# Narrower first and last chunks of tokens in a two-layer MLP pipeline

## The chip, the cores and the metric

The kernel runs on one core of one Trainium2 chip. The metric is the device time of one execution in microseconds. Before the change it is 1582.55 us, the median of 3 runs (1582.0 to 1582.71).

## What is computed

Attention over pooled keys, and behind it two MLPs. There are 12288 query tokens of 128 channels and 768 pooled keys; all tensors are float32.

```python
kv_pool = kv.reshape(B, H // r, r, W // r, r, C).mean(axis=(2, 4))
k = v = kv_pool.reshape(B, -1, C) @ w_sr
s = scale * (q @ k.transpose(0, 2, 1))
a = softmax(s)                    # with 1e-9 in the denominator
x = a @ v                         # 12288 x 128
# MLP 1 (d_ff = 2048)
h = x @ w_in1;  x = (maximum(h, 0) ** 2) @ w_out1
# MLP 2 (d_ff = 2048): a rational function of h
h = x @ w_in2
P = a[0] + a[1]*h + a[2]*h**2 + a[3]*h**3
Q = 1.0 + abs(b[0])*abs(h) + abs(b[1])*h**2
out = (P / (Q + 1e-6)) @ w_out2
```

## The kernel before, in words

Channels lie on the 128 partitions and tokens along the free dimension, so x is a tile `X` of 128 x 12288 that stays in the on-chip memory from the attention to the end. The tokens are cut into `NCH` = 24 chunks of `T` = 512.

The attention stage (`step_a`, L154 and its callers) is done first, for all tokens. The change leaves it as it is. It ends about 297.6 us after the start of the span.

The MLP stage is one long loop, written out step by step, that every engine walks in its own order. A step is numbered `s`. The 2048 hidden features are `NF` = 16 blocks of 128, so a unit of work `t` is one block of one chunk: `t // NF` is its chunk, `t % NF` its block, and `NB` = 24 x 16 = 384 units make up each MLP. `LAG` = 21 is the number of steps by which MLP 2 runs behind MLP 1, since MLP 2 needs a whole chunk of MLP 1's output. The loop has `STEPS` = 384 + 21 + 6 steps. In step s:

- TensorE (PE) does, in this order: **H2**, three float32r matmuls for unit s-21 of MLP 2 (`three`, L534 to L538: high and low parts of weights and of x); **H1**, three for unit s of MLP 1; **ACC1**, one float32 matmul for unit s-2 that adds the squared block into the output of MLP 1 (L637); **ACC2**, the same for unit s-25 of MLP 2 (L646). A float32 matmul shows in the trace as two records.
- ScalarE (ACT): the square of unit s-2 where it is even (L372), `abs` (L377) and the product with a[3] (L378) of unit s-21, the logarithm (L384) of unit s-22, the `Relu` of unit s (L392), and the exponential (L398) of unit s-22. At chunk ends it also takes the accumulators out of PSUM: `x2h` (L359) and the output `osb` (L366). In steps 2 to 5 it rounds the four parts of `win2h` (L333).
- VectorE (DVE): five `scalar_tensor_tensor` instructions per unit: L502, L508, L513, L519, L526; of these L502, L513 and L526 belong to unit s-23, L508 to unit s-22 and L519 to unit s-21. At chunk ends it also makes `x1h` (L485) and `x2l` (L493).
- GpSimd (POOL): two instructions for unit s-21 (L278, L280) and the square of unit s where it is odd (L286). In steps 6 to 9 it makes the four parts of `win2l` (L245), and in the steps with s % 16 = 9 the next chunk's `x1l` (L261).

So steps 0 to 20 hold work of MLP 1 alone, steps 21 to 383 work of both, and from step 384 on work of MLP 2 alone. H1 has two PSUM buffers and H2 has four, so H2 of unit t waits until L526 of unit t-4 is done (`need(pe, g2_rdy, t - H2_RING + 1)`). Nothing is reordered at run time: every engine's list is fixed in the program, and semaphores hold an engine at its next instruction until its inputs are there. SyncE (SP) issues one output DMA for each chunk.

Of the kernel before, what the change touches and what calls it, by code (L numbers as in the profile page):

```python
# [30 lines left out]
def build_program(nc, qT, kvT, w_sr, w_in1, w_out1, w_in2, w_out2, coef_a, coef_b, outT):  # L31
# [25 lines left out]
    with ExitStack() as ctx:  # L57
# [234 lines left out]
        def _(act):  # L292
# [57 lines left out]
            for s in range(STEPS):  # L350
# [4 lines left out]
                if chunk_end(t):  # L355
# [3 lines left out]
                    nc.scalar.activation(x2h[:, c % 2, :], ACC1, ACT.Identity).then_inc(x2h_rdy, 1)  # L359

                t = s - LAG - 5
                if chunk_end(t):
# [3 lines left out]
                    nc.scalar.activation(osb[:, c % 2, :], ACC2, ACT.Copy, scale=-1.0).then_inc(o_rdy, 1)  # L366

                t = s - 2
                if in_b(t) and on_act(t):
# [2 lines left out]
                    nc.scalar.activation(g1[:, t % G_RING, :], r1[:, t % R_RING, :], ACT.Square).then_inc(sqa_rdy, 1)  # L372
# [300 lines left out]
```

## Time and profile before

| | |
|---|---|
| time, median of 3 | 1582.55 us |
| the profiled execution's own time | 1581.61 us |
| its span, first to last instruction | 1579.8 us |
| mean granted TensorE clock | 0.992 |
| busy over the span: PE, DVE, ACT, POOL | 95%, 94%, 86%, 72% |
| attention stage | 0 to 297.6 us |
| MLP stage, steps of MLP 1 alone | 297.6 to about 331.5 us |
| MLP stage, both | about 331.5 to about 1504 us |
| MLP stage, MLP 2 alone | to the end, 1579.8 us |

A busy share is the time in which an engine had at least one instruction recorded as running. Records of one engine overlap: a DVE instruction that is recorded with 0.74 us can be followed by the next one 0.66 us after its start. What an instruction costs in a full queue is therefore read as the distance from its start to the next start, here called its pitch, and not as its duration.

### The profile page before, as it was taken

What the parts mean: (1) busy time and instruction counts of PE and PEld (TensorE: products, weight loads), DVE (VectorE), ACT (ScalarE), POOL (GpSimd) and SP (SyncE); (2) the same over time, 40 slices, a digit from 0 to 9 for tenths busy, and PEclk for the clock granted to TensorE, in tenths of its full rate; (3) what the DMA queues carried; (4) which work ended last, traced back from release to release, by engine and by line L of the source; (5) the groups of instructions that cost most, each with busy time, mean ns of one, the idle gap of its engine ahead of it and who ended that gap; (6) DMA issues with size and microseconds to landing.
All of it is one profiled execution on the core that took longest, in us unless ns stands there. A gap on an engine that the chain in (4) does not pass through costs nothing.

```text
span 1579.8 us, 20254 instructions
## 1 busy us (share of the span) xinstructions
PE 1505.4 (95%) x5452; PEld 963.9 (61%) x5452; DVE 1483.9 (94%) x2591; ACT 1354.6 (86%) x2581; POOL 1141.0 (72%) x1119
## 2 busy tenths in 40 slices
PE   5999999999999999999999999999999999999975
PEld 4899999655555555555555555555555555555532
DVE  7888888359999999999999999999999999999998
ACT  3776777679999999999999999999999999999975
POOL 2544444467888878887888788878888788878864
PEclk9999999999999999999999999999999999999988
DMA  5100003000000000000000000000000000000000
GB/s 214 28 20 27 20 27 100 0 1 1 7 7 8 7 1 7 7 7 1 7 7 7 1 7 8 7 1 8 7 7 7 1 7 7 8 1 7 7 7 7
DMA packets 11223, 24.39 MB, mean 15 GB/s; under 512 B 1408, under 2 KB 1536, under 8 KB 10880
## 3 DMA queue, kind: packets, MB, share of 16 engines
q1 hardware_dynamic: 11136, 23.40, 4.4%
q8 instruction: 33, 0.54, 0.1%
q14 instruction: 54, 0.44, 0.1%
HBM read 17.11 MB, written 6.29 MB: 15 GB/s over the span
## 4 chain that ended last, share of the span: by engine, by line
DVE 69%; PE 19%; issue 10%; ACT 1%; POOL 1%; DMA 0%; SPq 0%; DVEq 0%; POOLq 0%; ACTq 0%
DVE tb L526 19%; DVE tb L508 16%; DVE tb L502 16%; DVE psum L513 15%; PE psum L596 6%; PE psum L571 6%; PE psum L582 4%; DVE tb L519 1%; DVE x2l L493 1%; PE psum L637 1%; DMA X<-kvT 0%; DVE x1h L485 0%; PE psum L555 0%; POOL pnorm L238 0%; PE psum L646 0%
## 5 line engine op out<-in xcount | busy, mean ns | idle before, releaser
L280 POOL TENSOR_TENSOR wb<-wb,ub 128x512 f32<-128x512 f32 x384 | 493.9, 1286 | 32.1
L278 POOL TENSOR_SCALAR wb<-ub,babs 128x512 f32<-128x512 f32 x384 | 297.7, 775 | 205.5 <-ACT ub L377 203.8
L637 PE MATMUL psum<-g,wout 128*128 128x512 f32 x768 | 403.8, 608 | 27.7 <-DVE x2l L493 25.1
L646 PE MATMUL psum<-tb,wout 128*128 128x512 f32 x768 | 398.2, 601 | 5.5 <-DVE tb L526 4.0
L519 DVE SCALAR_TENSOR_TENSOR tb<-tb,ca,psum 128x512 f32<-128x512 f32 x384 | 328.1, 854 | 7.0 <-ACT tb L378 7.0
L508 DVE SCALAR_TENSOR_TENSOR tb<-tb,ca,psum 128x512 f32<-128x512 f32 x384 | 328.0, 854 | 0.0
L502 DVE SCALAR_TENSOR_TENSOR tb<-tb,ca,psum 128x512 f32<-128x512 f32 x384 | 326.9, 851 | 0.1
L536 PE MATMUL psum<-x2h,win2h 128*128 128x512 f32 x384 | 302.4, 788 | 19.2 <-DVE tb L526 19.2
L513 DVE SCALAR_TENSOR_TENSOR psum<-wb,psum 128x512 f32<-128x512 f32 x384 | 307.8, 802 | 0.0
L526 DVE SCALAR_TENSOR_TENSOR tb<-psum,tb 128x512 f32<-128x512 f32 x384 | 305.9, 797 | 0.2
L377 ACT ACTIVATE ub<-psum 128x512 f32<-128x512 f32 x384 | 226.6, 590 | 54.5 <-PE psum L538 53.9
L398 ACT ACTIVATE psum<-lnb 128x512 f32<-128x512 f32 x384 | 232.3, 605 | 44.4 <-DVE tb L508 40.7
L378 ACT ACTIVATE tb<-psum,ca 128x512 f32<-128x512 f32 x384 | 261.4, 681 | 0.0
L646 PEld LDWEIGHTS psum<-tb,wout 128*128 128x128 f32 x768 | 147.3, 192 | 185.1 <-issue 170.1
L384 ACT ACTIVATE lnb<-wb 128x512 f32<-128x512 f32 x384 | 242.0, 630 | 0.0
L392 ACT ACTIVATE r<-psum 128x512 f32<-128x512 f32 x384 | 229.3, 597 | 13.1 <-PE psum L538 13.1
L286 POOL TENSOR_TENSOR g<-r 128x512 f32<-128x512 f32 x192 | 200.2, 1042 | 19.8 <-ACT r L392 19.8
L238 POOL TENSOR_SCALAR pnorm<-prob,stat 128x768 f32<-128x768 f32 x96 | 87.2, 908 | 143.9 <-DVE stat L454 143.8
L637 PEld LDWEIGHTS psum<-g,wout 128*128 128x128 f32 x768 | 134.6, 189 | 89.2 <-DVE x2l L493 35.1
L536 PE MATMUL psum<-x1h,win1h 128*128 128x512 f32 x384 | 158.4, 413 | 0.1
L538 PE MATMUL psum<-x2h,win2l 128*128 128x512 f32 x384 | 153.1, 399 | 0.0
L537 PE MATMUL psum<-x2l,win2h 128*128 128x512 f32 x384 | 152.9, 398 | 0.0
(64 smaller groups left out, 2147.3 us busy)
## 6 DMA issues: line engine op xcount, KB each, us to landing
qraw<-qT SPq DMA_DIRECT2D x25, 256.0 KB, 2.6
X<-kvT SPq DMA_DIRECT2D x16, 384.0 KB, 7.6
outT<-osb SPq DMA_DIRECT2D x24, 256.0 KB, 2.0
wraw<-w_in SPq DMA_DIRECT2D x2, 1024.0 KB, 10.9
wsr<-w_sr SPq DMA_DIRECT2D x1, 64.0 KB, 1.9
wout<-w_out SPq DMA_DIRECT2D x2, 0.5 KB, 8.2
ca<-coef_a SPq DMA_DIRECT2D x1, 2.0 KB, 2.1
cb<-coef_b SPq DMA_DIRECT2D x1, 1.0 KB, 2.2
```

What stands on the lines that cost most here:

```text
L278: nc.gpsimd.tensor_scalar(w, u, babs[:, 1:2], babs[:, 0:1], ALU.mult, ALU.add).then_inc(v_rdy, 1)
L280: nc.gpsimd.tensor_tensor(w, w, u, ALU.mult).then_inc(w_rdy, 1)
L378: nc.scalar.activation(tb[:, t % T_RING, :], H2[t % H2_RING], ACT.Identity, scale=ca[:, 3:4]).then_inc(t1_rdy, 1)
L384: nc.scalar.activation(lnb[:, t % LN_RING, :], wb[:, t % W_RING, :], ACT.Ln, bias=Q_ONE).then_inc(ln_rdy, 1)
L502: nc.vector.scalar_tensor_tensor(out=y, in0=y, scalar=ca[:, 0:1], in1=r, op0=ALU.add, op1=ALU.mult).then_inc(y_rdy, 1)
L508: nc.vector.scalar_tensor_tensor(out=p, in0=p, scalar=ca[:, 1:2], in1=H2[t % H2_RING], op0=ALU.add, op1=ALU.mult).then_inc(t3_rdy, 1)
L513: nc.vector.scalar_tensor_tensor(out=r, in0=wb[:, t % W_RING, :], scalar=Q_ONE, in1=r, op0=ALU.add, op1=ALU.mult).then_inc(e_rdy, 1)
L519: nc.vector.scalar_tensor_tensor(out=p, in0=p, scalar=ca[:, 2:3], in1=H2[t % H2_RING], op0=ALU.add, op1=ALU.mult).then_inc(t2_rdy, 1)
L526: nc.vector.scalar_tensor_tensor(out=y, in0=H2[t % H2_RING], scalar=-2.0, in1=y, op0=ALU.add, op1=ALU.mult).then_inc(g2_rdy, 1)
L536: mm(out, lh, rh, start=start, stop=False)
L637: mm(ACC1, wout1[:, f, :], g1[:, t % G_RING, :], start=(f == 0), stop=(f == NF - 1))\
L646: mm(ACC2, wout2[:, f, :], tb[:, t % T_RING, :], start=(f == 0), stop=(f == NF - 1))\
```

## The change

The MLP stage gets a list of chunk widths `CW` and of their offsets `CO`. The first and the last chunk are 256 tokens wide, the 23 between are 512 wide; there are `NC` = 25 chunks and `NB` = 400 units per MLP. All 12288 tokens are still covered, since 256 + 23 x 512 + 256 = 12288. `LAG` stays 21. Every instruction of a unit works on `n = CW[t // NF]` columns of its buffer, and the buffers keep their size. The attention stage still makes chunks of 512, so chunk c of the MLP stage, which now begins 256 tokens earlier, waits for the attention chunk that holds its last token.

```diff
-    NB = NCH * NF
+    CW = [T // 2] + [T] * (NCH - 1) + [T // 2]
+    CO = [sum(CW[:c]) for c in range(len(CW))]
+    NC = len(CW)
+    NB = NC * NF
...
-            for c in range(NCH):
+            for c in range(NC):
                 sp.wait_ge(o_rdy, c + 1)
-                sp.dma_start(outT[:, c * T:(c + 1) * T], osb[:, c % 2, :]).then_inc(o_out[c % 2], 16)
+                sp.dma_start(outT[:, CO[c]:CO[c] + CW[c]], osb[:, c % 2, 0:CW[c]]).then_inc(o_out[c % 2], 16)
...
-                nc.gpsimd.tensor_tensor(x1l[:, c % 2, :], X[:, c * T:(c + 1) * T], x1h[:, c % 2, :].bitcast(F32),
+                n = CW[c]
+                nc.gpsimd.tensor_tensor(x1l[:, c % 2, 0:n], X[:, CO[c]:CO[c] + n], x1h[:, c % 2, 0:n].bitcast(F32),
                                         ALU.subtract).then_inc(x1_rdy, 1)
...
                 if in_b(t) and not on_act(t):
-                    r = r1[:, t % R_RING, :]
+                    n = CW[t // NF]
+                    r = r1[:, t % R_RING, 0:n]
                     pool.wait_ge(r1_rdy, t + 1)
                     need(pool, g1_used, t - G_RING + 1)
-                    nc.gpsimd.tensor_tensor(g1[:, t % G_RING, :], r, r, ALU.mult).then_inc(sqp_rdy, 1)
+                    nc.gpsimd.tensor_tensor(g1[:, t % G_RING, 0:n], r, r, ALU.mult).then_inc(sqp_rdy, 1)
...
-                dve.wait_ge(x_rdy, c + 1)
+                dve.wait_ge(x_rdy, -(-(CO[c] + CW[c]) // T))
...
                 t = s - LAG - 2
                 if in_b(t):
-                    y = tb[:, t % T_RING, :]
+                    n = CW[t // NF]
+                    y = tb[:, t % T_RING, 0:n]
                     dve.wait_ge(y_rdy, t + 1)
                     dve.wait_ge(e_rdy, t + 1)
-                    nc.vector.scalar_tensor_tensor(out=y, in0=H2[t % H2_RING], scalar=-2.0, in1=y,
+                    nc.vector.scalar_tensor_tensor(out=y, in0=H2[t % H2_RING][:, 0:n], scalar=-2.0, in1=y,
                                                    op0=ALU.add, op1=ALU.mult).then_inc(g2_rdy, 1)
...
-                    three(H2[t % H2_RING], win2h[:, f:f + P], win2l[:, f:f + P],
-                          x2h[:, c % 2, :], x2l[:, c % 2, :]).then_inc(h2_rdy, 1)
+                    three(H2[t % H2_RING][:, 0:n], win2h[:, f:f + P], win2l[:, f:f + P],
+                          x2h[:, c % 2, 0:n], x2l[:, c % 2, 0:n]).then_inc(h2_rdy, 1)
```

All other instructions of the units on ACT, DVE, POOL and PE are narrowed in the same way.

On POOL, this is the list of steps 0 to 14, where MLP 1 runs alone. `g` is the square of an odd unit, `win2l` a part of MLP 2's weights, `x1l` the low part of the next chunk's x. Before:

```order
L261 TENSOR_TENSOR x1l<-X,x1h 128x512
L286 TENSOR_TENSOR g_83<-r_82 128x512 x3
L245 TENSOR_TENSOR win2l<-wraw,win2h 128x512
L286 TENSOR_TENSOR g_83<-r_82 128x512
L245 TENSOR_TENSOR win2l<-wraw,win2h 128x512 x2
L261 TENSOR_TENSOR x1l<-X,x1h 128x512
L286 TENSOR_TENSOR g_83<-r_82 128x512
L245 TENSOR_TENSOR win2l<-wraw,win2h 128x512
```

The same place on POOL after:

```order
L265 TENSOR_TENSOR x1l<-X,x1h 128x256
L292 TENSOR_TENSOR g_83<-r_82 128x256 x3
L248 TENSOR_TENSOR win2l<-wraw,win2h 128x512
L292 TENSOR_TENSOR g_83<-r_82 128x256
L248 TENSOR_TENSOR win2l<-wraw,win2h 128x512 x2
L265 TENSOR_TENSOR x1l<-X,x1h 128x512
L292 TENSOR_TENSOR g_83<-r_82 128x256
L248 TENSOR_TENSOR win2l<-wraw,win2h 128x512
```

The order is the same; the squares are 256 wide, the weight parts and the second chunk's `x1l` are as wide as before.

On PE, this is step 25, in which all four kinds of matmul appear for the first time. Before:

```order
L536 MATMUL psum<-x2h_84,win2h_52 128x512
L537 MATMUL psum<-x2l_85,win2h_52 128x512
L538 MATMUL psum<-x2h_84,win2l_53 128x512
L536 MATMUL psum<-x1h_60,win1h_50 128x512
L537 MATMUL psum<-x1l_61,win1h_50 128x512
L538 MATMUL psum<-x1h_60,win1l_51 128x512
L637 MATMUL psum<-g1_83,wout1_54 128x512
L646 MATMUL psum<-tb_81,wout2_55 128x512
```

The same step on PE after:

```order
L554 MATMUL psum<-x2h_84,win2h_52 128x256
L555 MATMUL psum<-x2l_85,win2h_52 128x256
L556 MATMUL psum<-x2h_84,win2l_53 128x256
L554 MATMUL psum<-x1h_60,win1h_50 128x512
L555 MATMUL psum<-x1l_61,win1h_50 128x512
L556 MATMUL psum<-x1h_60,win1l_51 128x512
L658 MATMUL psum<-g1_83,wout1_54 128x512
L668 MATMUL psum<-tb_81,wout2_55 128x256
```

In steps 21 to 36 the matmuls of MLP 2 belong to the narrow first chunk, while those of MLP 1 belong to 512-wide chunks (from step 16 on; ACC1, which is two steps behind, from step 18 on).

On DVE, the instructions of the last two units at the end of the program before, and then after:

```order
L508 SCALAR_TENSOR_TENSOR tb_81<-tb_81,ca_57,psum 128x512
L513 SCALAR_TENSOR_TENSOR psum<-wb_79,psum 128x512
L526 SCALAR_TENSOR_TENSOR tb_81<-psum,tb_81 128x512
L502 SCALAR_TENSOR_TENSOR tb_81<-tb_81,ca_57,psum 128x512
L513 SCALAR_TENSOR_TENSOR psum<-wb_79,psum 128x512
L526 SCALAR_TENSOR_TENSOR tb_81<-psum,tb_81 128x512
```

```order
L523 SCALAR_TENSOR_TENSOR tb_81<-tb_81,ca_57,psum 128x256
L529 SCALAR_TENSOR_TENSOR psum<-wb_79,psum 128x256
L544 SCALAR_TENSOR_TENSOR tb_81<-psum,tb_81 128x256
L516 SCALAR_TENSOR_TENSOR tb_81<-tb_81,ca_57,psum 128x256
L529 SCALAR_TENSOR_TENSOR psum<-wb_79,psum 128x256
L544 SCALAR_TENSOR_TENSOR tb_81<-psum,tb_81 128x256
```

The last 16 units are 256 wide, and 16 units of five instructions have come in over the whole list.

## Rows read from the trace of the kernel before

**Rows 1.** The chain that ended last, from the page: shares of the span by engine:

```profile
DVE 69%; PE 19%; issue 10%; ACT 1%; POOL 1%; DMA 0%; SPq 0%; DVEq 0%; POOLq 0%; ACTq 0%
```

**Rows 2.** Busy time by stretch (window, length, busy us and instructions per engine, clock, DMA):

```profile
297.60:334.00 36.40, 34.43 (x111) 20.18 (x109) 0.69 (x1) 21.91 (x40) 16.98 (x16) 1.00 0.00 0
...
334.00:1516.00 1182.00, 1152.10 (x3644) 678.23 (x3643) 1181.14 (x1874) 1101.81 (x2057) 964.50 (x939) 1.00 0.02 6
```

**Rows 3.** Timeline of DVE, one step (start, duration, engine, line, instruction, idle before):

```profile
340.95 0.74 DVE L502 SCALAR_TENSOR_TENSOR tb<-tb,ca,psum 128x512 f32<-128x512 f32 x1
...
342.26 0.69 DVE L513 SCALAR_TENSOR_TENSOR psum<-wb,psum 128x512 f32<-128x512 f32 x1
...
342.86 0.74 DVE L519 SCALAR_TENSOR_TENSOR tb<-tb,ca,psum 128x512 f32<-128x512 f32 x1
...
344.12 0.73 DVE L502 SCALAR_TENSOR_TENSOR tb<-tb,ca,psum 128x512 f32<-128x512 f32 x1
```

**Rows 4.** Timeline of PE, start of the MLP stage, MLP 1 alone:

```profile
297.57 0.40 PE L536 MATMUL psum<-x1h,win1h 128*128 128x512 f32 x1
...
306.14 1.02 PE L637 MATMUL psum<-g,wout 128*128 128x512 f32 x2
...
307.23 0.40 PE L537 MATMUL psum<-x1l,win1h 128*128 128x512 f32 x1
...
307.70 1.02 PE L637 MATMUL psum<-g,wout 128*128 128x512 f32 x2
...
331.50 0.80 PE L536 MATMUL psum<-x2h,win2h 128*128 128x512 f32 x1
```

**Rows 5.** Timeline of DVE, its first unit and its seventeenth:

```profile
334.01 0.75 DVE L519 SCALAR_TENSOR_TENSOR tb<-tb,ca,psum 128x512 f32<-128x512 f32 x1 [6.24 <-ACT tb L378]
...
384.66 0.75 DVE L519 SCALAR_TENSOR_TENSOR tb<-tb,ca,psum 128x512 f32<-128x512 f32 x1
```

**Rows 6.** Timeline of POOL, steps 7 to 11 (parts of win2l, x1l, squares):

```profile
311.12 2.51 POOL L245 TENSOR_TENSOR win2l<-wraw,win2h 128x512 fp32r<-128x512 f32 x2
...
314.83 1.03 POOL L286 TENSOR_TENSOR g<-r 128x512 f32<-128x512 f32 x1
```

**Rows 7.** Groups of instructions by line and shape: busy us, mean ns | idle before:

```profile
L280 POOL TENSOR_TENSOR wb<-wb,ub 128x512 f32<-128x512 f32 x384 | 493.9, 1286 | 32.1
...
L278 POOL TENSOR_SCALAR wb<-ub,babs 128x512 f32<-128x512 f32 x384 | 297.7, 775 | 205.5 <-ACT ub L377 203.8
...
L311 ACT ACTIVATE pth<-psum 128x384 fp32r<-128x384 f32 x192 | 84.0, 489 | 76.1 <-PE psum L582 76.0
...
L359 ACT ACTIVATE x2h<-psum 128x512 fp32r<-128x512 f32 x24 | 14.0, 582 | 0.3 <-PE psum L637 0.3
```

**Rows 8.** Timeline of PE in the attention stage, narrower matmuls (128x384, 128x128):

```profile
283.88 0.51 PE L571 MATMUL psum<-kh,ql 128*128 128x384 f32 x2
284.23 0.82 PE L582 MATMUL psum<-ident,pnorm 128*128 128x128 f32 x6
284.80 0.48 PE L596 MATMUL psum<-pth,vh 128*128 128x512 f32 x1
```

**Rows 9.** Timeline of DVE ahead of the attention stage, narrower instructions:

```profile
18.66 0.55 DVE L412 TENSOR_TENSOR kl<-psum,kh 128x384 fp32r<-128x384 f32 x1
...
19.12 0.55 DVE L415 TENSOR_TENSOR vl<-psum,vh 128x384 fp32r<-128x384 f32 x1
```

**Rows 10.** Busy time by stretch, near the end, MLP 2 alone:

```profile
1510.00:1512.00 2.00, 0.80 (x2) 0.00 (x0) 2.00 (x5) 1.13 (x3) 0.93 (x1) 1.00 0.00 0
...
1516.00:1518.00 2.00, 1.99 (x4) 1.49 (x5) 2.00 (x4) 1.04 (x3) 1.31 (x2) 0.50 0.00 0
```

**Rows 11.** Timeline of all engines, the last two rows that set the end:

```profile
1573.83 0.69 DVE L526 SCALAR_TENSOR_TENSOR tb<-psum,tb 128x512 f32<-128x512 f32 x1
...
1576.68 0.60 ACT L366 ACTIVATE osb<-psum 128x512 f32<-128x512 f32 x1 [4.99 <-PE psum L646]
```

More of the change, by code:

```diff
@@ L270, in _ @@
             for s in range(STEPS):
-                if s % NF == 9 and s // NF + 1 < NCH:
+                if s % NF == 9 and s // NF + 1 < NC:
                     split_x1(s // NF + 1)
@@ L358, in _ @@
                     need(act, h2_rdy, (c - 1) * NF)
-                    nc.scalar.activation(x2h[:, c % 2, :], ACC1, ACT.Identity).then_inc(x2h_rdy, 1)
+                    nc.scalar.activation(x2h[:, c % 2, 0:CW[c]], ACC1[:, 0:CW[c]], ACT.Identity).then_inc(x2h_rdy, 1)
                 t = s - LAG - 5
@@ L365, in _ @@
                     need(act, o_out[c % 2], c // 2 * 16)
-                    nc.scalar.activation(osb[:, c % 2, :], ACC2, ACT.Copy, scale=-1.0).then_inc(o_rdy, 1)
+                    nc.scalar.activation(osb[:, c % 2, 0:CW[c]], ACC2[:, 0:CW[c]], ACT.Copy, scale=-1.0).then_inc(o_rdy, 1)
                 t = s - 2
@@ L371, in _ @@
                     need(act, g1_used, t - G_RING + 1)
[L372 removed]
+                    n = CW[t // NF]
+                    nc.scalar.activation(g1[:, t % G_RING, 0:n], r1[:, t % R_RING, 0:n], ACT.Square).then_inc(sqa_rdy, 1)
                 t = s - LAG
@@ L383, in _ @@
                     act.wait_ge(w_rdy, t + 1)
-                    nc.scalar.activation(lnb[:, t % LN_RING, :], wb[:, t % W_RING, :], ACT.Ln,
+                    n = CW[t // NF]
+                    nc.scalar.activation(lnb[:, t % LN_RING, 0:n], wb[:, t % W_RING, 0:n], ACT.Ln,
                                          bias=Q_ONE).then_inc(ln_rdy, 1)
@@ L397, in _ @@
                     act.wait_ge(ln_rdy, t + 1)
-                    nc.scalar.activation(H2[t % H2_RING], lnb[:, t % LN_RING, :], ACT.Exp,
+                    n = CW[t // NF]
+                    nc.scalar.activation(H2[t % H2_RING][:, 0:n], lnb[:, t % LN_RING, 0:n], ACT.Exp,
                                          scale=-1.0).then_inc(r_rdy, 1)
@@ L492, in _ @@
                     dve.wait_ge(x2h_rdy, c + 1)
-                    nc.vector.tensor_tensor(x2l[:, c % 2, :], ACC1, x2h[:, c % 2, :].bitcast(F32),
+                    n = CW[c]
+                    nc.vector.tensor_tensor(x2l[:, c % 2, 0:n], ACC1[:, 0:n], x2h[:, c % 2, 0:n].bitcast(F32),
                                             ALU.subtract).then_inc(x2_rdy, 1)
-                if s % NF == 7 and s // NF + 1 < NCH:
+                if s % NF == 7 and s // NF + 1 < NC:
                     split_x1(s // NF + 1)
@@ L625, in _ @@
                     need(pe, r1_rdy, t - H1_RING + 1)
-                    three(H1[t % H1_RING], win1h[:, f:f + P], win1l[:, f:f + P],
-                          x1h[:, c % 2, :], x1l[:, c % 2, :]).then_inc(h1_rdy, 1)
+                    three(H1[t % H1_RING][:, 0:n], win1h[:, f:f + P], win1l[:, f:f + P],
+                          x1h[:, c % 2, 0:n], x1l[:, c % 2, 0:n]).then_inc(h1_rdy, 1)
                 t = s - 2
@@ L636, in _ @@
                     pe.wait_ge(sqa_rdy if on_act(t) else sqp_rdy, t // 2 + 1)
-                    mm(ACC1, wout1[:, f, :], g1[:, t % G_RING, :], start=(f == 0), stop=(f == NF - 1))\
+                    n = CW[t // NF]
+                    mm(ACC1[:, 0:n], wout1[:, f, :], g1[:, t % G_RING, 0:n], start=(f == 0), stop=(f == NF - 1))\
                         .then_inc(g1_used, 1)
@@ L645, in _ @@
                     pe.wait_ge(g2_rdy, t + 1)
-                    mm(ACC2, wout2[:, f, :], tb[:, t % T_RING, :], start=(f == 0), stop=(f == NF - 1))\
+                    n = CW[t // NF]
+                    mm(ACC2[:, 0:n], wout2[:, f, :], tb[:, t % T_RING, 0:n], start=(f == 0), stop=(f == NF - 1))\
                         .then_inc(g2_used, 1)
```

38 lines of the change are left out of this document (24 added, 14 removed).

## The prediction

> **What bounds the kernel now.** I read the page first: in the chain that ended last, DVE has 69% and PE 19% [rows 1]. A share over the whole span mixes stages, so next I read the busy time by stretch. The reader is to see two regimes there [rows 2]. From 297.6 to 334.0 DVE is busy for 0.69 us of 36.4 and PE for 34.4: while MLP 1 runs alone, PE sets the time. From 334 to 1516 DVE is busy for 1181.1 of 1182.0 us: from there on it never waits. The timeline of DVE gives the price of one step: from one L502 to the next 3.17 us, with five instructions in it [rows 3]. L502 and L508 together take 1.31, that is 0.655 each (L519 alike), and L513 takes 0.60 (L526 alike); 3 x 0.655 + 2 x 0.60 = 3.17. PE alone takes 307.70 - 306.14 = 1.56 us for a step with one H1 and one ACC1 [rows 4]. From L637 to L537 is 1.09, a float32 matmul and one float32r matmul; two float32r ones take 0.47. So a float32r matmul of 512 columns costs 0.235 and a float32 one 0.86. A step with all four kinds is 3.12 us of PE against 3.17 of DVE. The two are nearly even in the middle, and only DVE's price counts there. No wait is worth removing in the middle; what can move is the fill, the drain, and the number of instructions.
>
> I call 297.57, the first H1 [rows 4], zero. H2 of unit 0 starts at 33.9 [rows 4]. DVE starts at 36.4, 2.5 later, and handles unit 16, the first of the second chunk, at 384.66 - 297.57 = 87.1 [rows 5]. From there both versions have the same 368 units of 512 columns, 3.17 us each, DVE without a gap. So the sum has four terms: when DVE reaches unit 16, the 16 new units behind the 368, the new chunk end, and the tail behind DVE.
>
> **Prices at 256 columns,** which the trace doesn't show.
> - DVE: two instructions at 384 columns start 0.46 apart [rows 9], the like at 512 takes 0.60, so 128 columns cost 0.14, about DVE's 1.04 ns per column. The rest, 0.07 (0.12 where a column of coefficients is read), stays: 0.655 - 0.267 = 0.39 and 0.33, a step 3 x 0.39 + 2 x 0.33 = 1.83. Bounds: 1.585 if all of it halved, 2.0 if each keeps 0.04 more.
> - PE: at 384 columns two float32r matmuls take 284.23 - 283.88 = 0.35, so 0.175 each; six of 128 columns, each with its own weights, take 0.57, so 0.095 each [rows 8]. A line through 512 and 384 gives 0.12 at 256; ends 0.107 (streaming alone) and 0.175 (as dear as 384). Float32: half of 0.86 and a little, 0.44. An H1 plus ACC1 step: 3 x 0.12 + 0.44 = 0.80.
> - POOL: L278 and L280 take 0.78 + 1.29 = 2.06 at 512 [rows 7]; at 256 between 1.03 and 2.06. I take 1.5; it stays under DVE's 1.83. A square costs 1.03 [rows 6], at 256 between 0.52 and 1.03; I take 0.60, near the lower end, since no POOL row shows a fixed part of more than a few tenths.
> - ACT: 582 - 489 = 93 ns per 128 columns [rows 7], so 0.19 per instruction. In the middle it is busy for 1101.8 us in some 366 steps [rows 2], 3.0 a step.
>
> **The fill, steps 0 to 20.** PE's own work falls: H1 16 x 0.36 + 5 x 0.70 = 9.3, ACC1 16 x 0.44 + 3 x 0.86 = 9.6, together 18.9 against 31.0 before (21 x 0.70 + 19 x 0.86). But POOL's list doesn't shrink with it: four `win2l` parts and the second chunk's `x1l` stay 512 wide, 1.24 us each ((314.83 - 311.12) / 3) [rows 6], all in steps 6 to 9. Before, they lay beside 1.56 us steps. Now PE comes to step 5 at about 3.2 of work + 1.4 of the same starting waits = 4.6, and POOL starts the square of unit 5 some 0.8 later, at 5.4. Then: square 0.60, part 1.24, square 0.60, parts 2.48, `x1l` 1.24, square of unit 9 0.60: 12.2. Another part and the square of unit 11: 14.0. ACC1 of unit 9 stands in step 11, where PE is at 4.6 + 6 x 0.80 + 0.36 = 9.8: it waits about 2.4 us, and everything on PE behind it waits too. From ACC1 of unit 11: 14.0 + 0.44, two narrow steps 1.6, two steps of a wide H1 and a narrow ACC1 2.3, step 18 with the wait for the first `x2l` 2.0, two wide steps 3.1. H2 of unit 0 starts at 23.4 instead of 33.9.
>
> **A clock term.** In the tail of before, PE was busy for 0.80 of 2.0 us and the granted clock then was 0.50, that is 1.2 instead of 2.4 GHz, in a stretch 4 us later [rows 10]. The new wait leaves a like hole in front of PE-bound work. I add 1.5 us: some 3 us of PE work at half speed. Bounds 0 and 3.4.
>
> **Steps 21 to 36, narrow MLP 2 beside wide MLP 1.** Before, DVE set 3.17. Now DVE needs only 1.83, but PE still has a wide H1 and ACC1: 0.36 + 0.70 + 0.86 = 1.92, and 0.44 more in the 12 steps with ACC2. That is 30.7 + 5.3 = 36.0. I add 0.7 for the chunk end in step 34, where ACC1 waits for `x2l` and no DVE backlog hides it any longer, and 0.5 for the start. H2 of unit 16 starts at 23.4 + 37.2 = 60.6, with the clock term 62.1, and DVE has it at 64.6 instead of 87.1: **-22.5**. ACT lies below: 3.0 - 4 x 0.19 = 2.25 a step. What is late next is PE, and DVE idles for some 9 us here. That is the heart of it: the half-width units save time on an engine that has nothing else to do in these steps.
>
> **The 16 new units.** DVE has them behind the 368: 16 x 1.83 = **+29.3**. Beside it lie PE (0.80 a step; 1.6 even at 1.2 GHz) and POOL (1.5). Seen over both ends, DVE does 32 narrow units for 16 wide ones: 58.6 for 50.7 us, 7.9 us of fixed cost.
>
> **The new chunk end.** One narrow `x1h` and one narrow `x2l` more on DVE: **+0.6**. Output DMAs: one more, hidden.
>
> **Behind DVE.** From L526's end, 1574.52, to `osb` at 1576.68 PE does one float32 matmul at the low clock [rows 10, 11]. Half the columns save about 0.9 there and 0.2 in `osb`, and the last transfer may gain 0.1: **-1.2**.
>
> Sum: -22.5 + 29.3 + 0.6 - 1.2 = +6.2. The profiled execution took 1581.6, 0.9 less than the median of 1582.55, so it becomes 1587.8, and the median 1588.8. I forecast 1588.8 us, **slower**; with its bounds 1586 to 1592.
>
> **A rule weighed.** PE's weight loads overlap its streaming in these rows: 0.235 for 512 columns leaves no room for a load beside 0.213 of streaming, and 128 columns with their load take 0.095 [rows 4, 8]. The Trainium skill (TensorE: Matmul & The Clock Gate, Part 3, The mechanism) says that a LDWEIGHTS overlaps matmuls in flight only when it goes to another row group, and gives 128 columns of weights about 107 ns; by it every narrow matmul would pay its load, which I estimate from that figure at some 9 us more. The rows of 512 and 384 columns speak against it, since their matmuls would have to show the same load.
>
> **Rivals.**
> - *The fill gives all it can* (not slower). It decides at POOL's list in steps 6 to 9: if squares and weight parts come through in time there (a square well below 0.60, parts started earlier because `win2h` is there early), PE never waits at step 11. H2 of unit 0 comes at 18.9 + 1.4 + 0.4 = 20.7, the clock stays, and if steps 21 to 36 have no waits either, the sum is 6.2 - 2.7 - 1.5 - 1.2 = +0.8: 1583.4, no change. For it: PE's floor really falls by 12 us. Against it: 1.24 x 5 us stand in POOL's list whatever the width. To come out faster by over 3.2 us, DVE's step at 256 would have to be under 1.6 as well, which [rows 9] speak against.
> - *The narrow step is set by POOL or ACT*. If L278 and L280 hardly shrink (2.06), the last 16 units cost 16 x 0.23 = 3.7 more and steps 21 to 36 up to 2.06 + 0.52 = 2.6 instead of 2.25, 5 more: 1597.5. For it: no POOL row has another width in the same form. Against it: POOL's L245, L261 and L280 all take 1.24 to 1.29 at 512, as work by the column would.
> - *A narrow matmul pays its load*. If the 0.095 of 128 columns is all load and comes on top at 256, the five loads of a step's narrow part (three for H2, two for ACC2) cost 5 x 0.08 = 0.4; 16 x 0.4 in steps 21 to 36 and 1.5 in the fill behind the POOL wait: 8 more, 1596.8. The tail hides it (1.2 under 1.83).
>
> **How the numbers follow.** Forecast and its bounds 0.60; fill gives all 0.20; POOL or ACT 0.12; loads 0.05; anything else, either way, 0.03. A difference below 0.2% (3.2 us) can't be told from none. Faster (under 1579.4) needs the first rival and a cheaper DVE at once: 0.06. Within 0.2% (to 1585.7): most of the first rival and the low edge of the forecast, 0.19. Slower: 0.75. The range 1583 to 1596 leaves out under 1 in 10 at each side.
>
> **What would show it.** Right: H2's first matmul about 23 to 25 us after the first H1, a PE wait of 2 to 3 us for a POOL square in step 11; in steps 21 to 36 DVE with idle time of some 9 us and PE without; a DVE step of 1.8 us in the last 16 units without idle time; wide steps in the middle unchanged at 3.17. Wrong: a DVE step at 256 columns below 1.6 or above 2.0, no PE wait in the fill, a PE step above 2.4 in steps 21 to 36, or a middle that differs from 3.17 per unit.

## The result, and the profile after

The changed kernel took 1586.49 us (median of 9 runs, 1585.51 to 1587.35), the kernel before 1581.47 (median of 9 beside them, 1581.22 to 1582.71). The ratio is 1.0031, with a 95% interval of 1.0022 to 1.0040: slower by 5.0 us. The forecast was 1588.8 us, slower, with 1583 to 1596 as the range. The profiled execution took 1585.51 us with a span of 1583.7 us and a mean TensorE clock of 0.994.

The chain of the changed kernel gives DVE less and waiting for issue more than [rows 1]:

```profile
DVE 66%; PE 19%; issue 12%; ACT 1%; POOL 1%; DMA 1%; SPq 0%; DVEq 0%; POOLq 0%; ACTq 0%
```

Times below are counted from the first H1, as in the prediction. It starts at 296.76 in this execution, at 297.57 in the one before [rows 4]. First the fill, the steps in which MLP 1 runs alone. The timeline of PE after (start, duration, instruction, idle before in brackets) has the first H1, the wait in step 11, H2 of unit 0 and H2 of unit 16, the first of a 512-wide chunk:

```profile
296.76 0.28 PE L554 MATMUL psum<-x1h,win1h 128*128 128x256 f32 x1
...
307.68 0.28 PE L556 MATMUL psum<-x1h,win1l 128*128 128x256 f32 x1
309.72 0.70 PE L658 MATMUL psum<-g,wout 128*128 128x256 f32 x2 [1.77 <-POOL g L292]
...
320.89 0.68 PE L554 MATMUL psum<-x2h,win2h 128*128 128x256 f32 x1
...
357.36 0.58 PE L554 MATMUL psum<-x2h,win2h 128*128 128x512 f32 x1
```

H2 of unit 0 starts at 24.1 instead of 33.9, H2 of unit 16 at 60.6. PE stands still for 1.77 us at the square of unit 9. The timeline of POOL over the same steps, against [rows 6], shows why: the squares have shrunk, the parts of `win2l` and the second chunk's `x1l` have not.

```profile
302.96 0.61 POOL L292 TENSOR_TENSOR g<-r 128x256 f32<-128x256 f32 x1 [1.74 <-PE psum L658]
303.53 1.28 POOL L248 TENSOR_TENSOR win2l<-wraw,win2h 128x512 fp32r<-128x512 f32 x1
304.80 0.61 POOL L292 TENSOR_TENSOR g<-r 128x256 f32<-128x256 f32 x1
305.37 2.52 POOL L248 TENSOR_TENSOR win2l<-wraw,win2h 128x512 fp32r<-128x512 f32 x2
307.84 1.26 POOL L265 TENSOR_TENSOR x1l<-X,x1h 128x512 fp32r<-128x512 f32 x1
309.06 0.61 POOL L292 TENSOR_TENSOR g<-r 128x256 f32<-128x256 f32 x1
```

Next steps 21 to 36. The windows of the changed kernel (length, then busy time of PE, PE weight loads, DVE, ACT, POOL, clock, DMA) have a third regime between the two of [rows 2]: from 322 to 360 PE is full and DVE is not. From 360 on DVE never waits, as before.

```profile
322.00:360.00 38.00, 37.89 (x158) 26.21 (x157) 31.79 (x79) 34.34 (x91) 30.52 (x43) 1.00 0.00 1
360.00:1500.00 1140.00, 1112.74 (x3541) 656.93 (x3540) 1139.86 (x1810) 1062.98 (x1989) 930.38 (x906) 1.00 0.02 6
```

One step of this regime on PE and on DVE. PE's pitch, from H2 to H2, is 335.90 - 333.56 = 2.34. DVE has the same pitch (338.49 - 336.14), with a pause in each step:

```profile
333.56 0.47 PE L554 MATMUL psum<-x2h,win2h 128*128 128x256 f32 x1
333.86 0.28 PE L555 MATMUL psum<-x2l,win2h 128*128 128x256 f32 x1
333.98 0.28 PE L556 MATMUL psum<-x2h,win2l 128*128 128x256 f32 x1
...
335.65 0.59 PE L668 MATMUL psum<-tb,wout 128*128 128x256 f32 x2
335.90 0.47 PE L554 MATMUL psum<-x2h,win2h 128*128 128x256 f32 x1
```

```profile
336.14 0.48 DVE L516 SCALAR_TENSOR_TENSOR tb<-tb,ca,psum 128x256 f32<-128x256 f32 x1 [0.25 <-ACT psum L410]
...
337.42 0.48 DVE L536 SCALAR_TENSOR_TENSOR tb<-tb,ca,psum 128x256 f32<-128x256 f32 x1
...
338.49 0.48 DVE L516 SCALAR_TENSOR_TENSOR tb<-tb,ca,psum 128x256 f32<-128x256 f32 x1 [0.25 <-ACT psum L410]
...
359.65 0.75 DVE L536 SCALAR_TENSOR_TENSOR tb<-tb,ca,psum 128x512 f32<-128x512 f32 x1 [0.83 <-ACT tb L387]
```

The last row is unit 16 on DVE, at 359.65 - 296.76 = 62.9, against 87.1 before [rows 5]: 24.2 us earlier.

In the middle nothing moved: from the `x2l` of one chunk to that of the next it takes 51.66 us on average, and 51.64 before. At the end, the timelines of DVE and of all engines:

```profile
1574.32 0.49 DVE L536 SCALAR_TENSOR_TENSOR tb<-tb,ca,psum 128x256 f32<-128x256 f32 x1
...
1576.16 0.49 DVE L536 SCALAR_TENSOR_TENSOR tb<-tb,ca,psum 128x256 f32<-128x256 f32 x1
...
1579.46 0.42 DVE L544 SCALAR_TENSOR_TENSOR tb<-psum,tb 128x256 f32<-128x256 f32 x1
1579.94 0.50 PEld L668 LDWEIGHTS psum<-tb,wout 128*128 128x128 f32 x2 [0.76 <-DVE tb L544]
1581.20 0.38 ACT L372 ACTIVATE osb<-psum 128x256 f32<-128x256 f32 x1 [3.01 <-PE psum L668]
```

DVE's narrow step is 1.84 us (1576.16 - 1574.32), without a pause. From unit 16 to the end of the last instruction of L544 it takes 1220.2 us, where the like took 1189.9 before: +30.4. Behind it there are 3.8 us to the end of the span instead of 5.3 [rows 11]: -1.5. Together -24.2 + 30.4 - 1.5 = +4.7. The span grew by 3.9 only, since the first H1 came 0.8 earlier, which the experiments below explain.

### The profile page after: what moved, and what is told of

Same layout as the page of the kernel before. It is cut to its first block, busy times and chain, and to the rows that moved or that the text cites. A ratio compares the mean times of both kernels' runs of the same rounds, so it can differ in the third digit from the quotient of the medians.

```text
span 1583.7 us, 20851 instructions
## 1 busy us (share of the span) xinstructions
PE 1508.5 (95%) x5612; PEld 979.3 (62%) x5612; DVE 1495.0 (94%) x2673; ACT 1363.9 (86%) x2671; POOL 1151.0 (73%) x1160
## 4 chain that ended last, share of the span: by engine, by line
DVE 66%; PE 19%; issue 12%; ACT 1%; POOL 1%; DMA 1%; SPq 0%; DVEq 0%; POOLq 0%; ACTq 0%
DVE tb L544 16%; DVE tb L523 16%; DVE tb L516 16%; DVE psum L529 14%; PE psum L614 6%; PE psum L589 6%; PE psum L600 4%; DVE tb L536 1%; PE psum L658 1%; DVE x2l L506 1%; DMA X<-kvT 1%; DVE x1h L497 1%; PE psum L668 0%; PE psum L555 0%; PE psum L556 0%
## 5 line engine op out<-in xcount | busy, mean ns | idle before, releaser
L285 POOL TENSOR_TENSOR wb<-wb,ub 128x512 f32<-128x512 f32 (+1 forms) x400 | 497.0, 1243 | 33.4
L283 POOL TENSOR_SCALAR wb<-ub,babs 128x512 f32<-128x512 f32 (+1 forms) x400 | 303.1, 758 | 209.0 <-ACT ub L386 207.1
L658 PE MATMUL psum<-g,wout 128*128 128x512 f32 (+1 forms) x800 | 407.5, 591 | 35.5 <-DVE x2l L506 25.1
L668 PE MATMUL psum<-tb,wout 128*128 128x512 f32 (+1 forms) x800 | 400.0, 582 | 3.4 <-DVE tb L544 2.9
L554 PE MATMUL psum<-x2h,win2h 128*128 128x512 f32 (+1 forms) x400 | 306.1, 765 | 13.6 <-DVE tb L544 13.6
L536 DVE SCALAR_TENSOR_TENSOR tb<-tb,ca,psum 128x512 f32<-128x512 f32 (+1 forms) x400 | 290.3, 726 | 8.0 <-ACT tb L387 7.3
L516 DVE SCALAR_TENSOR_TENSOR tb<-tb,ca,psum 128x512 f32<-128x512 f32 (+1 forms) x400 | 289.0, 722 | 2.5 <-ACT psum L410 2.5
L523 DVE SCALAR_TENSOR_TENSOR tb<-tb,ca,psum 128x512 f32<-128x512 f32 (+1 forms) x400 | 290.2, 726 | 0.0
L529 DVE SCALAR_TENSOR_TENSOR psum<-wb,psum 128x512 f32<-128x512 f32 (+1 forms) x400 | 269.0, 672 | 0.0
L544 DVE SCALAR_TENSOR_TENSOR tb<-psum,tb 128x512 f32<-128x512 f32 (+1 forms) x400 | 267.2, 668 | 0.2
L387 ACT ACTIVATE tb<-psum,ca 128x512 f32<-128x512 f32 (+1 forms) x400 | 265.5, 664 | 0.0
L394 ACT ACTIVATE lnb<-wb 128x512 f32<-128x512 f32 (+1 forms) x400 | 245.4, 613 | 0.0
L241 POOL TENSOR_SCALAR pnorm<-prob,stat 128x768 f32<-128x768 f32 x96 | 87.1, 908 | 142.9 <-DVE stat L466 142.6
L556 PE MATMUL psum<-x2h,win2l 128*128 128x512 f32 (+1 forms) x400 | 155.6, 389 | 0.0
L555 PE MATMUL psum<-x2l,win2h 128*128 128x512 f32 (+1 forms) x400 | 155.4, 389 | 0.0
```

Of the source, the lines that this page charges most:

```text
L283: nc.gpsimd.tensor_scalar(w, u, babs[:, 1:2], babs[:, 0:1], ALU.mult, ALU.add).then_inc(v_rdy, 1)
L285: nc.gpsimd.tensor_tensor(w, w, u, ALU.mult).then_inc(w_rdy, 1)
L387: nc.scalar.activation(tb[:, t % T_RING, 0:n], h, ACT.Identity, scale=ca[:, 3:4]).then_inc(t1_rdy, 1)
L394: nc.scalar.activation(lnb[:, t % LN_RING, 0:n], wb[:, t % W_RING, 0:n], ACT.Ln, bias=Q_ONE).then_inc(ln_rdy, 1)
L516: nc.vector.scalar_tensor_tensor(out=y, in0=y, scalar=ca[:, 0:1], in1=r, op0=ALU.add, op1=ALU.mult).then_inc(y_rdy, 1)
L523: nc.vector.scalar_tensor_tensor(out=p, in0=p, scalar=ca[:, 1:2], in1=h, op0=ALU.add, op1=ALU.mult).then_inc(t3_rdy, 1)
```

## The experiments

The kernel before was run beside each of them (medians of 1581.2 to 1581.5 us).

**The narrow chunks at one end alone.** `front2` has both at the start, `end2` both at the end.

```diff
-    CW = [T // 2] + [T] * (NCH - 1) + [T // 2]
+    CW = [T // 2] * 2 + [T] * (NCH - 1)         # front2
+    CW = [T] * (NCH - 1) + [T // 2] * 2         # end2
```

> Widths 256, 256 and 23 times 512: both narrow chunks in front. Theory A: H2 of unit 0 at about 24 us less 1.4 for the narrower steps 16 to 20 (some 22); steps 21 to 36 have both MLPs narrow, DVE sets 1.84 a step (29.4), steps 37 to 52 pair narrow MLP 2 with wide MLP 1, PE sets 2.34 (38 with the chunk end); the first 512-wide unit reaches DVE at about 92 to 93 instead of 87.1, and the tail behind DVE is the wide one of before (5.3 us): 6 to 7 us over the kernel before, ratio 1.004. Rival D (the cost is only the number of instructions and chunk ends, wherever they are): the same 5 us as the change, less its tail gain of 1.5, so 6.5 as well, but with the fill gain visible and no DVE idle time in steps 37 to 52. The idle time of DVE in steps 37 to 52 (some 8 us by A, none by D) tells them apart.

> Widths 23 times 512, 256, 256: both narrow chunks at the end. Theory A: the fill is that of before (H2 of unit 0 at 33.9, DVE at unit 16 at 87.1), 32 narrow units of 1.84 replace 16 wide ones of 3.17 on DVE, which never idles: +8.1, one narrow chunk end +0.6, tail -1.5: 7 us over the kernel before, ratio 1.0045; no DVE idle time anywhere after unit 0. So the change as made should beat this by 2 us: that is all that the shorter fill is worth net. Rival E (the fill gain is real and large, as an 11 us earlier start of DVE suggests): without it this version is some 12 us or more over before.

Measured: `front2` 1587.91 us, ratio 1.0038 (1.0024 to 1.0051); `end2` 1588.30 us, ratio 1.0041 (1.0027 to 1.0054). In `end2` the fill is that of the kernel before (H2 of unit 0 at 33.9 after the first H1), and the window of the middle has DVE full:

```profile
384.00:1520.00 1136.00, 1102.00 (x3526) 651.96 (x3525) 1136.00 (x1804) 1054.29 (x1982) 922.65 (x904) 1.00 0.02 6
```

So `end2` prices the splitting by itself: 32 narrow units for 16 wide ones, one more chunk end, and the shorter way behind DVE make +6.8. The changed kernel, +5.0, recovers only 1.8 of that with a fill that is 9.8 us shorter. `front2` shows the same from the other side. Its window with narrow MLP 2 units shows a full PE and a DVE with pauses:

```profile
350.00:388.00 38.00, 37.89 (x162) 26.89 (x161) 33.27 (x83) 34.19 (x92) 29.89 (x42) 1.00 0.01 5
```

DVE reaches the first wide unit, now unit 32, at 92.9 instead of 87.1. A first H2 at 21.5 and a longer PE-paced stretch behind it end up later than the kernel before. Theory A had expected some 8 us of idle time on DVE here, rival D none; the window shows 38.00 - 33.27 = 4.7, which speaks against D, though it is less than A had said. The total, +6.4, tells nothing between them.

**POOL's list in the fill.** `spread` puts the parts of `win2l` in steps 6, 11, 14 and 17 instead of 6 to 9.

```diff
-                if 6 <= s < 6 + W_PARTS:
-                    split_w(1, win2l, win2h, s - 6, wl_rdy)
+                if s in (6, 11, 14, 17):
+                    split_w(1, win2l, win2h, (6, 11, 14, 17).index(s), wl_rdy)
```

> The changed kernel with POOL's four win2l parts in steps 6, 11, 14 and 17 instead of 6 to 9. Theory A (the price is DVE's fixed cost of 16 more units plus DVE idling in steps 21 to 36, where PE sets 2.34 us a step): the 1.8 us PE wait for the square of unit 9 goes, H2 of unit 0 comes 1.8 us earlier, about 22.3 us after the first H1, nothing else moves; 1.8 us faster than the changed kernel, still some 3 us over the kernel before (ratio 1.002). Rival B (the held-up fill is what makes the change slower): most of the 5 us come back, ratio 1.000 or under. Rival C (the wait is only passed on, because ACT or the x2l chain is next): less than 0.5 us.

Measured: 1583.85 us, ratio 1.0014 (1.0005 to 1.0024). The same window of PE, length 6.00, first of the changed kernel and then of `spread`:

```profile
306.00:312.00 6.00, 4.23 (x25) 3.43 (x23) 0.00 (x0) 2.55 (x8) 5.47 (x6) 1.00 0.00 0
```

```profile
306.00:312.00 6.00, 6.00 (x34) 5.03 (x34) 0.00 (x0) 3.59 (x11) 4.78 (x6) 1.00 0.00 0
```

The wait is gone, and H2 of unit 0 comes at 22.3, 1.8 earlier; DVE has unit 16 at 61.1, also 1.8 earlier. Between the two profiled executions the gain is 1.8 us, between the medians 2.6; a difference of 0.8 is within the scatter that is described below. The first rival needed this list out of the way. With it gone the kernel is still slower, by 2.3 us.

**PE's share of steps 21 to 36.** `short_after` and `short_before` leave out one of the three matmuls of H1, `x1l` times `win1h`, in these 16 steps, in the changed kernel and in the one before. The output loses that term there.

```diff
-                mm(out, lh, rl, start=False, stop=False)
+                if not short:
+                    mm(out, lh, rl, start=False, stop=False)
...
-                          x1h[:, c % 2, 0:n], x1l[:, c % 2, 0:n]).then_inc(h1_rdy, 1)
+                          x1h[:, c % 2, 0:n], x1l[:, c % 2, 0:n], short=LAG <= s < LAG + NF).then_inc(h1_rdy, 1)
```

> The changed kernel with one of H1's three float32r matmuls (x1l times win1h) left out in steps 21 to 36 alone; that part of the product is missing from the output. Theory A (PE sets these steps at 2.34 us and DVE idles): each of 16 steps loses 0.235 us of PE, 3.8 in all if nothing comes next, 3 if ACT (about 2.1 a step) comes close behind: 1583.5 to 1582.7. Rival H (in these steps a latency loop through ACT's exponential and DVE's L516 sets the pace, as the 0.25 us waits of L516 for L410 suggest): less than 1 us.

> The kernel before with the same matmul left out in the same steps 21 to 36 (the same part of the product is missing). Theory A: DVE sets 3.17 us a step there without idle time, PE's shorter work is worth nothing, at most 0.5 us at the start of the stretch, where DVE's first units still wait: 1581 to 1581.5. If PE set the pace as in the changed kernel, it would gain 3.8.

Measured: `short_before` 1581.26 us, ratio 1.0 (0.999 to 1.0009). Where DVE paces, 16 x 0.235 us less on PE is worth nothing. `short_after` 1584.84 us, ratio 1.0023 (1.0014 to 1.0032): 1.7 less than the changed kernel in the medians, and DVE has unit 16 only 1.2 earlier, at 61.7. The expectation of 3 to 3.8 was a miss, and rival H, with less than 1, missed it from the other side. PE's timeline in `short_after` shows the next limit:

```profile
334.90 1.02 PE L659 MATMUL psum<-g,wout 128*128 128x512 f32 x2
...
337.36 1.13 PE L659 MATMUL psum<-g,wout 128*128 128x512 f32 x2 [0.17 <-ACT g L379]
...
339.57 1.02 PE L659 MATMUL psum<-g,wout 128*128 128x512 f32 x2
```

The mean step is (348.31 - 334.90) / 6 = 2.23 between ACC1 of seven steps, where PE's own work would be 2.34 - 0.235 = 2.11. The one wait that the trace names there is that for ACT's square. ACT itself isn't full (it pauses for 0.2 to 0.3 us in several of these steps), so this is a chain through ACT and not the sum of ACT's work, which the prediction had put at 2.25; which chain it is, the runs don't show. So PE paces this stretch at 2.34, as predicted, but the next limit stands only about 0.1 us behind it.

**Other widths.** `w384` is 384, 23 x 512, 128; `w128` is 128, 23 x 512, 384.

> Widths 384, 23 times 512, 128. Theory A, by the prices now measured: narrow H1 plus ACC1 1.17 us, H2 of unit 0 some 27.5 us after the first H1, steps 21 to 36 at PE's 2.7 (42.4 with chunk end and start), DVE at unit 16 at 72.4 instead of 87.1 (-14.7); 16 units of 128 columns at 1.2 to 1.4 us on DVE (+20.5), chunk end 0.5, tail -1.9: 4.4 us over the kernel before (3 to 6), ratio 1.003. Rival I (the cost falls with the width of the first chunk, since fill and steps 21 to 36 cancel, and the tail's gain is larger): under 2 us over before.

> The changed kernel with widths 128, 23 times 512, 384. Theory A: DVE reaches the first 512-wide unit some 57 to 58 us after the first H1 instead of 87.1 (minus 29 to 30; the second chunk is 512 wide and PE paces steps 16 to 36 as in the changed kernel), 16 more units of 384 tokens at 2.50 us each cost 40, one more chunk end 0.75, and the end behind DVE is 0.9 shorter: plus 9 us over the kernel before (7.5 to 11), 1590.5 us. Rival B: the narrower the first chunk the cheaper the change, because what is paid at the end is proportional to width while the fill is given back whole: 5 us or less over the kernel before.

Measured: `w384` 1585.64 us, ratio 1.0028 (1.0017 to 1.0039); `w128` 1593.03 us, ratio 1.0076 (1.0062 to 1.0090). The +4.4 of `w384` is what was expected, but not by the way that was expected: unit 16 comes at 73.4 instead of 72.4, and what follows is cheaper by nearly as much. The table sets the changed kernel between them; the times of unit 16 are counted from the first H1, the step is DVE's in the last 16 units.

| first, last width | H2 of unit 0 | unit 16 on DVE | gained at the front | last step | over before |
|---|---|---|---|---|---|
| 512, 512 | 33.9 | 87.1 | | 3.17 | |
| 384, 128 | 28.8 | 73.4 | 13.7 | 1.17 | +4.4 |
| 256, 256 | 24.1 | 62.9 | 24.2 | 1.84 | +5.0 |
| 128, 384 | 23.7 | 59.6 | 27.5 | 2.50 | +11.8 |

DVE's step is a straight line in the width, 0.50 + 0.667 per 128 columns. What a narrower front gives back falls off: 13.7, then 10.5, then 3.3 for each 128 columns, while each costs 16 x 0.667 = 10.7 at the end. For `w128` +9 was expected; 2.1 of the missing 2.8 us are there by unit 16. Its fill is hardly shorter than with 256. PE's timeline and the windows around the next row say why: a longer wait for the same POOL list, and this one has a clock of 0.50 behind it.

```profile
308.02 0.54 PE L658 MATMUL psum<-g,wout 128*128 128x128 f32 x2 [2.44 <-POOL g L292]
```

```profile
308.00:310.00 2.00, 1.98 (x11) 1.98 (x11) 0.00 (x0) 0.28 (x1) 1.56 (x2) 0.58 0.00 0
310.00:312.00 2.00, 2.00 (x11) 2.00 (x11) 0.00 (x0) 0.76 (x3) 0.40 (x1) 0.50 0.00 0
312.00:314.00 2.00, 2.00 (x8) 1.71 (x8) 0.00 (x0) 0.48 (x2) 0.40 (x1) 0.50 0.00 0
314.00:316.00 2.00, 2.00 (x10) 1.72 (x9) 0.00 (x0) 0.98 (x2) 0.00 (x0) 0.71 0.00 0
```

A PE step takes 1.07 us there (ACC1 at 309.96 and at 311.03), and 0.67 ahead of the wait. The rival, a change that is the cheaper the narrower its first chunk, is refuted. How much of the 2.1 us is the clock's was not measured by itself. PE's timeline of `w128` also shows that float32r matmuls hardly come closer below 256 columns: 0.11 apart at 128, against 0.12 at 256.

```profile
297.25 0.28 PE L554 MATMUL psum<-x1h,win1h 128*128 128x128 f32 x1
297.36 0.27 PE L555 MATMUL psum<-x1l,win1h 128*128 128x128 f32 x1
```

**The lag alone.** `lag19` and `lag18` are the kernel before, all chunks 512 wide, with another distance between MLP 1 and MLP 2. (The kernel before has `NF + 5`; where the expectation of `lag18` says `NF+4` that is a slip.)

```diff
-    LAG = NF + 5
+    LAG = NF + 3         # lag19
+    LAG = NF + 2         # lag18
```

> The kernel before (24 chunks of 512) with LAG = NF + 3 instead of NF + 5: MLP 2 starts two steps earlier. Theory F: in the fill PE sets 1.56 us a step and DVE has nothing to do, so two steps fewer bring DVE's start forward by 3.1 us and shorten the program by 3.1; in the middle x2l is done before PE reaches H2 of the next chunk (x2l ends 1.4 us before that H2 in the trace of before at LAG 21), so nothing new waits: 3.1 us faster, ratio 0.998. Rival G: H2 of each chunk's first unit now waits for x2l and DVE has a hole at each of 24 chunk ends: from 0.2 us each on it is slower than before.

> The kernel before (24 chunks of 512) with the second matmul stage one step earlier again: LAG is NF+2 instead of NF+4. The run with NF+3 gave 1578.5 us against 1581.5. Theory A: the fill is shorter by another 1.0 to 1.6 us, but the H2 of each chunk's first unit now stands in PE's order in the step in which DVE only begins to make x2l, so that PE waits for it at each of the 23 chunk ends; with DVE always full behind it, every such hole above DVE's backlog of about 1 us is paid, 0.5 to 1 us each, so that the time is 1588 to 1600 us. Rival B: the backlog hides the wait and only the fill counts: 1577.0 us.

Measured: `lag19` 1578.49 us (median of 11), ratio 0.9982 (0.9973 to 0.9991): 3.0 us faster than the kernel before, and the fastest of all. H2 of unit 0 comes 3.1 earlier, two PE steps of 1.56. `lag18` 1627.74 us, ratio 1.0296 (1.0282 to 1.0310). The sums of PE's waits from the start of MLP 2 to 1500 (waiter, what it waits for: total, times, longest) tell the two apart, first `lag19`, then `lag18`:

```profile
PE psum L637 <- DVE x2l L493: 24.4, 22, 1.1
PE psum L637 <- ACT g L372: 1.2, 2, 0.8
```

```profile
PE psum L536 <- DVE x2l L493: 47.4, 21, 2.5
PE psum L637 <- ACT g L372: 0.9, 1, 0.9
```

In `lag19`, as in the kernel before (24.4 too), it is ACC1 that waits 1.1 us for `x2l` at each chunk end, with the H2 that DVE needs next already done, and DVE doesn't notice. In `lag18` H2 itself waits for `x2l`, up to 2.5 us at 21 chunk ends, and DVE then waits for ACT's product of that unit:

```profile
DVE tb L519 <- ACT tb L378: 28.7, 38, 1.3
```

Behind most of these holes the granted clock falls too, as the rows of one chunk end show (PE's timeline, then the window behind it); over the middle it is 0.97 instead of 1.00.

```profile
485.66 0.53 PE L536 MATMUL psum<-x2h,win2h 128*128 128x512 f32 x1 [2.19 <-DVE x2l L493]
```

```profile
486.00:488.00 2.00, 2.00 (x6) 1.62 (x5) 1.52 (x3) 0.92 (x2) 0.22 (x1) 0.50 0.00 0
```

But it doesn't fall behind all of them. Here is another chunk end of `lag18`, with a longer wait and the clock at 1.00:

```profile
433.04 0.50 PE L536 MATMUL psum<-x2h,win2h 128*128 128x512 f32 x1 [2.27 <-DVE x2l L493]
```

```profile
434.00:436.00 2.00, 2.00 (x9) 1.15 (x7) 1.65 (x4) 1.95 (x4) 1.17 (x2) 1.00 0.04 8
```

The sign was as theory A had it, the size was far above its 0.5 to 1 us a chunk: 49 us over `lag19` is 2.1 for each of 23 chunk ends. The trace splits this in two. From the `x2l` of one chunk to the next it takes 51.67 us in `lag19`. In `lag18` it takes 52.6 where the clock stays at 1.00, so the hole alone costs 1.0, the upper end of what theory A had said. Where the clock falls it takes 54.2 to 54.3, so the clock costs another 1.6. Of the 23 chunk ends 18 have it. More than half of the 49 us is therefore the clock, which the expectation had left out.

**Both together.** `spread_lag19` is the changed kernel with `LAG = NF + 3` and the parts of `win2l` in steps 6, 11, 14 and 16.

> The changed kernel with POOL's win2l parts in steps 6, 11, 14 and 16 and LAG = NF + 3. Theory A: the two savings add up, 2.6 us from the POOL list (measured) and 3.0 from two steps less of fill (measured on the kernel before): 1580.8, a little under the kernel before and 2.3 us over the kernel before with LAG = NF + 3 alone. Rival J (a shorter fill leaves POOL or the x2l chain in the way again): 1582 or more.

Measured: 1580.23 us (1580.8 was expected), ratio 0.9994 (0.9985 to 1.0003), so it can't be told from the kernel before. It is the fastest of the variants with narrow chunks, and `lag19` without narrow chunks is 1.7 us faster.

**Two more profiles of the changed kernel.** Its nine runs lie in two groups, 1585.5 to 1585.6 and 1586.3 to 1587.4.

> The changed kernel once more, for one more profiled execution. Its times fell in two groups, 1585.5 to 1585.6 us and 1586.3 to 1587.4 us, and the profiled one belongs to the first. Theory A: in the second group PE's granted clock falls to 0.5 for some us behind the 1.8 us in which it waits for POOL's square in step 11, and the first H2 comes 1 to 2 us later than the 24.1 us after the first H1 of the profiled one, with the time up by as much. Rival B: the first H2 comes at 24.1 us in either group, and the extra lies ahead of the first H1 or behind the last unit.

> The changed kernel a third time, for one more profiled execution, with the same two theories as for the second: A, a time of 1586.3 us or more goes with a granted clock of 0.5 behind PE's wait in step 11 and a first H2 later than 24.1 us after the first H1; B, the extra lies ahead of the first H1 or behind the last unit.

Measured: 1586.84 and 1586.56 us, both of the upper group. Theory A was wrong, and its rival B held. H2 of unit 0 comes 24.1 after the first H1 in all three executions, unit 16 on DVE at 62.9 in all three, and the clock is 1.00 behind the POOL wait. The extra lies ahead of the first H1, which starts at 298.07 and 297.79 instead of 296.76. The windows show where, in the first matmuls of the attention stage. The same 20 us, first of the profiled execution of the changed kernel, then of `again1`:

```profile
20.00:40.00 20.00, 14.75 (x83) 11.51 (x82) 15.63 (x41) 11.05 (x24) 8.79 (x9) 1.00 0.23 86
```

```profile
20.00:40.00 20.00, 16.39 (x81) 13.08 (x79) 14.99 (x38) 10.36 (x22) 7.50 (x8) 0.91 0.26 93
```

A short drop of the clock there (mean 0.91 over 20 us) goes with 1.0 to 1.3 us. The profiled execution of the kernel before has it too (0.91, first H1 at 297.57). It comes or stays away whichever kernel runs: of the 14 profiled executions of this case, six have 0.91 in these 20 us and a first H1 between 297.6 and 298.2, the other eight have 1.00 and a first H1 between 296.7 and 297.3. It is all that separates the three profiled executions of the changed kernel; that it also separates the two groups of its other runs is likely and not shown. With the drop in both, the changed kernel's 1586.56 and 1586.84 stand against 1581.61: +5.0 to +5.2, of which the first H1 has 0.2 to 0.5 and the MLP stage +4.7, the sum read above.

## Why the prediction was right

The direction, the mechanism and nearly every term held. The total is closer than the terms, since some of their errors cancel.

- *What bounds.* PE in the fill and in steps 21 to 36, DVE from then on: right. The middle is unchanged to 0.02 us per chunk.
- *Prices at 256 columns.* DVE's step 1.84 (predicted 1.83, a line through the rows of 384 and 512 columns). PE: float32r 0.12 (`L555` to `L556` above), float32 0.43 (0.25 from its start to the H2 behind it, and that H2's first matmul takes 0.30 instead of 0.12), a step of H1 and ACC1 0.79 where it isn't held (0.80). POOL: a square 0.61 (0.60), and L283 and L285 1.33 together (1.5).
- *The fill.* H2 of unit 0 at 24.1 (23.4). The wait in step 11 is where it was said to be, but 1.77 long instead of 2.4. POOL starts the square of unit 5 at 302.96 - 296.76 = 6.2 instead of 5.4, and all that hangs on its list is 0.8 later: the release at 13.0 instead of 12.2, and H2 of unit 0. PE came to step 11 at 11.2 instead of 9.8. Half of that is its pair of steps, which takes 1.83 there and not 1.6, because each second ACC1 starts 0.15 late. The timeline names no wait, but in each pair this ACC1, of an even unit, starts 0.05 us after ACT's square of that unit ends, as here (ACT, then PE):

```profile
304.61 0.41 ACT L379 ACTIVATE g<-r 128x256 f32<-128x256 f32 x1
```

```profile
305.08 0.70 PE L658 MATMUL psum<-g,wout 128*128 128x256 f32 x2
```

So ACT's square, by these times, holds the narrow fill above PE's own work, and this goes on in `spread` (pairs of 1.83 as well), where POOL no longer does. The prediction had no term for it.

- *The clock term.* This is the term that failed: +1.5 us for a granted clock of 0.50 behind that wait. It stayed at 1.00 in all three profiles of the changed kernel, behind a wait of 1.77. In `w128`, with a wait of 2.44, it did fall, for some 7 us, and unit 16 came 2.1 later than expected without it. So such a drop exists, but that the length of the wait decides is not shown: in `lag18` five of 23 waits of 2.2 to 2.8 us left the clock at 1.00. The size of 1.5 had no row behind it either: where the clock fell, it stayed low for some 7 us in `w128` and for some 3 to 4 in `lag18`. The term makes most of the difference between predicted -22.5 and measured -24.2.
- *Steps 21 to 36.* PE's step 2.34, the sum of 1.92 and 0.44 (2.36); H2 of unit 16 at 60.6 (60.6 without the clock term). That this agrees to the tenth is luck: H2 of unit 0 came 0.7 later than predicted, and the way from there to unit 16 took 36.5 instead of 37.2. DVE idles for less than predicted. Between its units 0 and 16, 37.0 us, it is busy for 31.4, so 5.6 us are idle (9): the 2.34 - 1.84 = 0.50 of a step come only in the twelve steps with ACC2, since PE's step is 1.91 in the first four. The chunk end shows there too: `x2l` waits 0.77 us for ACT's `x2h`, since no backlog covers it.
- *The 16 new units, the chunk end.* +30.4 together (+29.9).
- *Behind DVE.* -1.5 (-1.2).
- *The base.* The three runs known beforehand had a median of 1582.55; over nine runs, these three among them, it was 1581.47. The early clock drop may be why, but these runs have no trace, and the profiled execution, which has the drop, took 1581.61. This moved the predicted time by 1.1 us and not the predicted difference: forecast +6.2, measured +5.0.
- *The range.* Its upper end of 1596 was said to leave out under 1 in 10, but the two rivals that were reckoned at 1597.5 and 1596.8 had 0.17 between them. This didn't matter for the result.

Of the rivals, *the fill gives all it can* was half true: `spread` gives it 1.8 us more, and it still isn't enough, because the price of the splitting (6.8 us, by `end2`) doesn't depend on the fill. Even then H2 of unit 0 came at 22.3 and not at the 20.7 of that rival. *POOL or ACT sets the narrow step* was wrong in price (POOL 1.33), though a chain through ACT is closer to PE there than I wrote. *A narrow matmul pays its load* was wrong at 256 columns: each matmul has a load of its own, and they start 0.12 apart, half of the 0.235 at 512, so hardly anything fixed comes on top. At 128 columns, by `w128`, this no longer holds: 0.11 is nearly twice what half of 0.12 would be.

The rule that was weighed (the Trainium skill, TensorE: Matmul & The Clock Gate, Part 3, The mechanism), that a load overlaps only when it goes to another row group, would have put some 9 us on top, by the prediction's estimate. The trace disagrees: PE's step in steps 21 to 36 is 2.34 us, which is the sum of the pitches of its matmuls and leaves nothing for five loads of the narrow part. The same section also names the background weight buffer as a target of loads that are pulled ahead, which the prediction left out; with that sentence the trace doesn't conflict.
